# A fused attention and two-MLP kernel: the vector engine's and GpSimd's work around changes of weights is put in another order

## The reference

```python
kv = einsum('bhsd,bhse->bhde', k, v);  out = einsum('bhsd,bhde->bhse', q, kv)
x  = (out / sqrt(mean(out*out, -1) + 1e-6) * g_norm)      # 8 batches, 8 heads, 576 x 64
x  = x.transpose(0, 2, 1, 3).reshape(4608, 512)
x  = (sigmoid(x @ w_gate) * (x @ w_val)) @ w_out          # layer 0: d_model 512, d_ff 1536
x  = (silu(x @ w2_gate) * (x @ w2_val)) @ w2_out          # layer 1, the same sizes
```

## Time and profile before

| | us |
|---|---|
| three runs, median (lowest to highest) | 1764.64 (1764.11 to 1765.32) |
| the profiled execution's own time | 1764.99 |
| its span, from first to last instruction | 1762.5 |
| PE busy in the span | 1726.5 (98%) |
| DVE busy | 1217.5 (69%) |
| ACT busy | 891.7 (51%) |
| POOL busy | 372.6 (21%) |
| mean granted TensorE clock | 0.996 |

### The profile page before, as it was taken

How to read it: one execution, slowest core, us unless ns; L and a number is a source line. 1 busy time by engine, 2 the same in 40 slices (tenths; PEclk the granted TensorE clock), 3 DMA queues, 4 the chain that set the end, 5 groups by cost and what they waited for, 6 DMA issues and landing times.

```text
span 1762.5 us, 30827 instructions
## 1 busy us (share of the span) xinstructions
PE 1726.5 (98%) x11182; PEld 1690.8 (96%) x11182; DVE 1217.5 (69%) x1937; ACT 891.7 (51%) x1708; POOL 372.6 (21%) x326
## 2 busy tenths in 40 slices
PE   9999999999999999999998999999999999999998
PEld 7899899999999999999998999999999999999998
DVE  4977677787666678666678777787666668655555
ACT  5766565655444445444445555565444445544444
POOL 5722222031111143111143000013111124111111
PEclk9999999999999999999999999999999999999999
DMA  9887786586555576555565455566555566555553
GB/s 238 253 286 197 263 265 175 211 298 221 197 198 197 198 243 223 198 197 197 197 192 186 179 197 197 200 248 222 204 202 198 197 227 217 172 187 188 183 186 93
DMA packets 200214, 366.92 MB, mean 208 GB/s; under 512 B 50048, under 2 KB 160128, under 8 KB 200064
## 3 DMA queue, kind: packets, MB, share of 16 engines
q1 hardware_dynamic: 200064, 364.96, 61.7%
HBM read 234.36 MB, written 130.55 MB: 207 GB/s over the span
## 4 chain that ended last, share of the span: by engine, by line
PE 76%; DVE 5%; issue 2%; POOL 1%; SPq 0%; ACT 0%; DMA 0%; DVEq 0%; ACTq 0%
PE ps L811 74%; DVE hop L1305 1%; PE ps L753 1%; DVE arena L1355 1%; DVE arena L1373 1%; DVE wb L1211 1%; DVE arena L1317 0%; DVE arena L1322 0%; DMA wops<-in_moe_w_out_dram 0%; DVE wa L1211 0%; SPq L434 0%; DVE xo L1216 0%; PE ps L673 0%; ACT wa L864 0%; SPq L453 0%
## 5 line engine op out<-in xcount | busy, mean ns | idle before, releaser
L811 PE MATMUL ps<-xo,wa 128*128 128x384 f32 x6048 | 1081.3, 337 | 5.7 <-ACT arena L1008 2.1
L811 PEld LDWEIGHTS ps<-xo,wa 128*128 128x128 f32 x6048 | 1049.6, 188 | 10.5 <-issue 4.3
L1008 ACT ACTIVATE arena<-ps 128x384 f32<-128x384 f32 x648 | 317.6, 491 | 576.4 <-PE ps L811 574.6
L1355 DVE TENSOR_TENSOR arena<-ps,arena 128x384 f32<-128x384 f32 x648 | 351.6, 553 | 368.1 <-PE ps L811 292.0
L811 PE MATMUL ps<-hop,wb 128*128 128x384 f32 x3024 | 541.0, 336 | 12.6 <-DVE hop L1305 8.6
L811 PEld LDWEIGHTS ps<-hop,wb 128*128 128x128 f32 x3024 | 523.0, 188 | 19.3 <-DVE hop L1305 10.9
L1305 DVE TENSOR_TENSOR hop<-arena,hop 128x384 fp32r<-128x384 f32 (+1 forms) x396 | 286.9, 748 | 31.7 <-ACT hop L990 25.8
L1614 POOL TENSOR_TENSOR arena<-arena 128x384 f32<-128x384 f32 x144 | 146.2, 1038 | 752.3 <-DVE arena L1355 752.3
L990 ACT ACTIVATE hop<-arena 128x384 fp32r<-128x384 f32 (+1 forms) x396 | 233.4, 608 | 80.7 <-DVE arena L1373 43.6
L1022 ACT ACTIVATE arena<-arena 128x384 f32<-128x384 f32 x216 | 112.6, 521 | 63.0 <-DVE arena L1355 62.9
L1373 DVE TENSOR_TENSOR arena<-arena 128x384 f32<-128x384 f32 x216 | 127.8, 593 | 20.3 <-DVE arena L1355 1.4
(11 more groups left out here) (72 smaller groups left out, 797.1 us busy)
## 6 DMA issues: line engine op xcount, KB each, us to landing
xo<-x_operands SPq DMA_DIRECT2D x168, 768.0 KB, 6.1
x_operands<-xo SPq DMA_DIRECT2D x84, 768.0 KB, 5.2
x<-arena SPq DMA_DIRECT2D x120, 384.0 KB, 3.2
arena<-x SPq DMA_DIRECT2D x96, 384.0 KB, 4.6
xraw<-x SPq DMA_DIRECT2D x22, 768.0 KB, 6.0
wops<-in_moe_w_gate_dram SPq DMA_DIRECT2D x24, 256.0 KB, 4.6
wops<-in_moe_w_val_dram SPq DMA_DIRECT2D x24, 256.0 KB, 4.5
wops<-in_moe_w_out_dram SPq DMA_DIRECT2D x48, 128.0 KB, 2.3
```

Of the source, the lines that this page charges most:

```text
L811: mm = pe.matmul(dst, lhsT, rhs, start=(pr in (1, 5, 2) and c == 0 and i == 0), stop=(c == 1 and i == 2), skip_group_check=(pr in (6, 7, 4 ...
L1008: nc.scalar.activation(dst, X(side), ACT.Copy).then_inc(copied, 1)
L1355: nc.vector.tensor_tensor(dst, acc, buf, ALU.add).then_inc(summed, 1)
```

## The change

It has four parts.

1. POOL: in the last block of a pass, the differences of units 2 and 3 of the next pass wait for the semaphore of hop_split(4). Where p > 0 (qq = 11, 17, 29), those of unit 3 also come after the six partial additions.
2. In the first block of a pass, window 1, the SUMMED part of unit 5 is split later, on ACT behind gated(22), on DVE behind hidden(22).
3. The tokens of qq = 18 are loaded in window 2 of qq = 16, and DVE's x_s1_s3 for it is done at the start of qq = 17. For qq = 18 and 19 DVE's split_x(2) and its store go from window 1 to window 2 of the block before. For qq above 18 x_s1_s3 is done behind total(22, 1) instead of ahead of it.
4. SP: in qq = 18 the loads of units 4 and 5 go ahead of most of the stores of the prepared tokens.

```diff
+        LEAP = NPASS * NB
+        def second_late(qq):
+            return awaits(qq, 0) or qq in (LEAP, LEAP + 1)
...
 # sync, window 0
-                    if first_pass(qq):
+                    if qq == LEAP:
+                        load_w(6 * (qq // NB) + 4)
+                        store_xo(qq, X_ORDER[4])
+                        store_xo(qq, X_ORDER[5])
+                        load_xraw(nxt, 0)
+                        load_w(6 * (qq // NB) + 5)
+                        store_xo(qq, X_ORDER[6])
+                    elif first_pass(qq):
                         for pr in X_ORDER[2 if awaits(qq, 1) else 4:]:
                             store_xo(qq, pr)
-                    if blk == 0 and qq > 0:
+                    if blk == 0 and qq != LEAP:
                         load_w(6 * (qq // NB) + 4)
                         load_w(6 * (qq // NB) + 5)
...
-                    if prepares and l == 1:
+                    if prepares and l == 1 and blk > 0:
                         load_xraw(nxt, 0)
 # sync, windows 1 and 2
-                    if early_x and l == 0:
+                    if early_x and l == 0 and p == 0:
                         load_xraw(nxt, 0)
...
-                    if early_x:
+                    if early_x and not second_late(nxt):
                         store_xo(nxt, X_ORDER[1])
...
-                if prepares and l == 0 and not awaits(nxt, 1):
+                if prepares and l == 0 and p == 0 and not awaits(nxt, 1):
                     load_xraw(nxt, 1)
+                if qq + 2 == LEAP:
+                    for t in range(2):
+                        load_xraw(LEAP, t)
...
-                if prepares and awaits(nxt, 0):
+                if prepares and second_late(nxt):
                     store_xo(nxt, X_ORDER[1])
 # scalar, window 1 of a pass's first block
-                                    for part in (RAW, SUMMED):
-                                        split_w(6 * (qq // NB) + 5, part)
+                                    split_w(6 * (qq // NB) + 5, RAW)
...
                             if w < 2:
                                 gated(22)
+                            if w == 1 and blk == 0 and qq > 0:
+                                split_w(6 * (qq // NB) + 5, SUMMED)
 # vector, windows 0 and 1
+                        if w == 0 and nxt == LEAP:
+                            x_s1_s3(nxt)
...
-                        if units:
+                        if units and (blk > 0 or w == 0):
                             for part in (RAW, SUMMED):
                                 split_w(units[1], part)
+                        elif units:
+                            split_w(units[1], RAW)
...
                         hidden(22)
+                        if units and blk == 0 and w == 1:
+                            split_w(units[1], SUMMED)
                         if is_late(u + 1):
                             unit_norm(u + 1)
-                        if w == 1 and prepares and not awaits(nxt, 0):
+                        if w == 1 and prepares and not second_late(nxt):
                             split_x(nxt, 2)
 # vector, window 2
-                        if prepares and awaits(nxt, 0):
+                        if prepares and second_late(nxt):
                             split_x(nxt, 2)
                         total(22, 0)
...
                         early_x = prepares and not awaits(nxt, 1)
-                        if early_x:
+                        if early_x and nxt < LEAP:
                             x_s1_s3(nxt)
                         total(22, 1)
+                        if early_x and nxt > LEAP:
+                            x_s1_s3(nxt)
 # gpsimd
                 if first_unit is not None:
+                    pool.wait_ge(hop_lo, n_hop(qq, 4, None))
                     differences(first_unit + 2)
-                    differences(first_unit + 3)
+                    if p == 0:
+                        differences(first_unit + 3)
                 if p > 0:
                     ...  # the six additions
+                    if first_unit is not None:
+                        differences(first_unit + 3)
```

## The result

| | before | after |
|---|---|---|
| median (lowest to highest), runs | 1764.38 (1763.53 to 1765.32), 4 | 1748.62 (1747.26 to 1749.68), 4 |
| ratio, 95% interval | 1 | 0.991 [0.9893, 0.9927] |
| profiled execution: time / span / granted clock | 1764.99 / 1762.5 / 0.996 | 1747.73 / 1745.3 / 0.998 |

What follows compares the result with a forecast made beforehand. TensorE, busy 98%, bounds the kernel; its losses at pass ends and the layer change were put mainly to VectorE's hop splits, slowed by POOL. 1764.99 - 9.3 + 1.5 - 7.0 = 1750.2, stated as 1750; range 1745 to 1757.

Steps and rivals of the forecast that it cites:

- the four ends: Last blocks of passes (5, 11, 23, 29): hop splits run quicker without POOL beside them; 9.3 us gained, 8 to 9.9.
- the leap: Change of layer, blocks 17 and 18: 7.0 us gained together, between 3 and 12.
- Blocks 12 and 30: First blocks of passes: POOL's moved differences come late and slow VectorE's split of unit 2; +0.75 us each, 0 to 2.
- Part 2: Later SUMMED split of unit 5 in first blocks of passes: 0, within 0.15 us either way, in each of four blocks.
- The leap up to block 18's first matmul: Four terms up to that matmul: hop stretch -1.8, split_x(2) -0.9, token sums -2.6, split_x(2) returning +1.3; sum -4.0 us.
- POOL out of the hop stretch: Block 17's hop splits run without POOL's work beside them: -1.8 us.
- Behind that matmul: Rest of block 18: clock -2.6, window 1 waits -1.9, split_x(2) of block 19 -0.9, POOL's differences +2.4; sum -3.0 us.
- slower: POOL falls behind: Rival: POOL's additions at 1.67 us delay ScalarE's copy; 8.4 us lost in each of blocks 12, 18, 30; 1773.7; 4%.
- whole instructions: Rival: moved differences cost VectorE four times 1.05; 2 us more in each of blocks 12, 18, 30; 1756.2; 6%.
- Little from the leap: Rival: VectorE's list bounds blocks 17 and 18 and work only shifts within it; 2.5 us gained there; 1754.7; 20%.
- the leap whole: Rival: clock stays, ScalarE's wait goes, differences fit into pauses; 12 us gained in blocks 17 and 18; 1745.2; 16%.
- Doesn't do what it says: Rival: hop splits stay slow for another reason, only 3 to 5 us won at the layer change; 1760 to 1762; 8%.

Runs made afterwards that it cites:

- e1: The kernel before with GpSimd's (POOL's) part of the change alone; 1750.22 us, ratio 0.9917.
- e2: The changed kernel with GpSimd's part undone, all other parts kept; 1758.25 us, ratio 0.9964.
- e3: The kernel before, with POOL's differences of units 2 and 3 of each later pass cut to 2 columns per block, order unchanged; 1756.5 us, one run.
- e6: The changed kernel with part 2 undone: SUMMED of unit 5 split together with RAW again; 1750.97 us, one run.
- e7: The changed kernel with the token sums x_s1 and x_s3 for block 18 back in window 2 of block 17; 1747.44 us, one run.
- e5: The changed kernel, with POOL in block 17 making unit 3's differences before the six additions; 1746.73 us, one run.
- e11: The changed kernel unaltered, run again; 1749.72 us, ratio 0.9914.
- e4: The changed kernel, with the SUMMED split of unit 3 later in window 0 of block 18, on ScalarE and VectorE; 1746.39 us, ratio 0.9892.
- e8: The changed kernel; in block 17 POOL makes unit 2's differences without waiting for hop splits, unit 3's behind them, before the additions; 1745.74 us, ratio 0.9893.
- e9: The changed kernel, with the SUMMED halves of units 3 and 5 split late in block 18 only; 1744.18 us, ratio 0.9884.

## Why the prediction was right, by its steps

The total was right (1748.6 for 1750), and so was what carries most of it, the four ends. Of the leap the sum was right (-7.7 for -7.0) and its parts were not: 1.5 us too little was counted ahead of block 18's first matmul and 0.8 too much behind it, and that these partly cancel was luck.

- **The four ends, -9.3:** measured -9.49. The hop splits run at 1.02 for two, as read from block 6; e1 and e2 show that it is GpSimd's part, and e3 that it is POOL's time and not another wait. Right in mechanism and size.
- **Blocks 12 and 30, +0.75 each:** measured +0.04 and +0.34. The chain was right in kind and counted too high. ScalarE did not wait: the differences of unit 3 ended at +7.9, the early end of the range given. The slower split of unit 2 (2.75; 1.0 more was counted, 0.7 came) shifted unit 4's load (POOL begins on it at 10.1 us, for 9.6 before) and VectorE's list, as forecast, and this reached TensorE in w1: 15.1 to 15.2 us in both blocks in all eleven runs with GpSimd's part, 14.8 in the three without. So it costs 0.3 in each. Not forecast was what came back in w0, 14.56 with the part and 14.71 and 14.81 before; why is not settled. With GpSimd's part alone (e1) block 12 is 0.27 faster than before and block 30 is 0.23 slower. Part 2's cost comes on top.
- **Part 2, 0 within 0.15 in each of four blocks:** measured about 0.2 in each, +0.9 in all, just outside. At the leap it was counted under ScalarE's wait, with 1.9; e6 has 2.2 to 3.4 us for it.
- **The leap up to block 18's first matmul, -4.0:** measured -5.54. POOL out of the hop stretch was under-counted: -1.8 was forecast, and GpSimd's part alone took 3.16 from w2 (e1), where e3, which leaves the additions where they were, took 2.36. The rest of the change gave 1.63 by itself (e2) and the last 0.75 only together with GpSimd's part. The two sums of tokens were counted with 2.6, and e7 has 3.3. For the split_x(2) out of window 1 (-0.9) the trace speaks, though no run moves it alone: the wait of 1.25 at 918.68 is there in e1 (1.26) and e3 (1.25) and gone in the kernel after and in e2. Its cost at the new place (+1.3) was not tested.
- **Behind that matmul, -3.0:** measured -2.18, and made up otherwise than forecast. ScalarE's wait in w1 went, and w1 fell by 3.1 (forecast 1.9). The split_x(2) of block 19 gave 1.4 in w2 (forecast 0.9), if all of w2's gain is put to it; TensorE's wait of 1.45 for VectorE at the start of w2 went, and it stands in e1 and e3 (1.46), but no run moves this piece alone. Nor has part 4, SyncE's order, a run of its own. But w0 grew by 2.3 where the forecast for it, +2.4 for POOL's differences less 2.6 for the clock, comes to -0.2. The clock's loss went from 2.6 (18 matmuls in 5.69) to 1.9, where the step had it go to nothing. The rest is TensorE's wait of 3.17 for the copy of product 7: the +2.4 priced POOL's late differences by what they cost VectorE's list, and what they cost was a wait in ScalarE's.

That wait is the mechanism of the rival "slower: POOL falls behind", which was priced at 8.4 us in each of blocks 12, 18 and 30 with additions at 1.67. It came at block 18 alone, with additions at 1.59: POOL was done at +12.6, not +17.4, and TensorE lost 3.2 there. In 12 and 30 the additions took 0.98, as the prediction argued against it. The rival "whole instructions" (four times 1.05) also fell where it was put: VectorE's two instructions on unit 2 in block 12 lost 0.7 together. This does not speak against the lock, as the prediction read the earlier trace rows: the second waits for what is left of the first, which is rarely the whole (see the last section). "Little from the leap" and "the leap whole" lie on both sides of the -7.72 measured. "Doesn't do what it says" fell with blocks 5 to 29.

What was expected to be seen: the four ends at 43.69 to 44.03 (one of them 0.03 outside the 43.7 to 44.0 given), POOL idle until the fourth hop split, and block 19 untouched at 43.68. Blocks 19 to 22 stayed at 43.68 each, so x_s1_s3 behind total(22, 1) cost nothing, as taken. Seen otherwise: block 12 at 44.60 without waits at slots 10 to 13 of w0; an idle time of 0.58 for 1.2 at block 18's start; ScalarE's wait over 2 us for POOL, in block 18 and not in 12 or 30. Blocks 17 and 18 took 94.62 for 95.3.

Not settled: why GpSimd's part and the others give 0.75 more together in w2 of block 17 than one by one (e1 and e2 have one profiled execution each), and why the low clock comes after some waits and not after others (below).

## What to carry to other kernels

Where an engine that isn't the bound slows one that is through the memory they share, move its work behind the critical stretch, and then follow its list to the end: what stands behind the move is late, and who waits for it may hold something else. Here a copy that TensorE needed stood in ScalarE's list behind a split that waited for GpSimd; putting the copy first was worth 1.9 to 2.5 us, part of it clock. Before moving a piece in every pass, ask at which place it pays: part 2 gave 2.2 to 3.4 us at one place and cost 0.9 at four.

## What the runs showed of the hardware that was not expected

- When GpSimd and a VectorE instruction with both operands in SBUF meet, the second pays, and what it pays is what is left of the first less about 0.14 us. In the traces of the kernels before and after, from block 5 on, 55 meetings are of one instruction with one other alone. Where 0.98 us was left the second took 0.84 to 0.85 longer, where 0.55 was left 0.41 to 0.42, where 0.29 was left 0.15. POOL's difference of 0.74 takes 1.46 beside a hop split that keeps its 0.96; VectorE's L1280 of 0.96 takes 1.76 beside POOL's additions, and those 1.59 for 0.98. VectorE's totals, which read PSUM and one buffer, stay at 0.54 to 0.56 beside the same additions.
- TensorE's clock. In the kernel after, TensorE idled 3.17 us and then ran at 1.2 GHz for a while, with 22 matmuls in 5.69 us; after the 0.58 us at the start of the block nothing fell. The length of the wait doesn't decide it. The clock fell at waits of 2.06 (e3, e7), 2.07, 2.08 (e1), 2.11 (e2), 2.66 (e5) and 3.17 us (after, e11). It stayed at 1.00 after another wait of 2.08 in e1 and after one of 3.17 in e6. In e1 (timeline, and the windows of both places):

```profile
931.39 14.89 PE L811 MATMUL ps<-xo,wa 128*128 128x384 f32 x75 [2.08 <-issue]
...
961.46 4.83 PE L811 MATMUL ps<-xo,wa 128*128 128x384 f32 x24 [2.08 <-ACT arena L1008]
```

```profile
959.50:963.00 3.50, 1.54 (x9) 1.00 0.76 244
931.20:935.80 4.60, 4.41 (x16) 0.63 0.47 187
```

  Behind the first the granted clock was 0.63 over 4.6 us, behind the second 1.00. No wait of 1.9 us or less in blocks 5 to 35 was followed by a fall; in e4, e8 and e9 none at the leap exceeds 1.05 us. What decides above that, these runs don't tell.
